# The first expert's rows are transposed ahead of the second search's counts, and that search's first levels move into the expert's phase

## The reference

```python
def _moe2_ref(x, w_gate, w1, w2) -> np.ndarray:
    N, D = x.shape                 # 3072, 384
    E = w_gate.shape[1]            # 8
    cap = N // E                   # 384
    logits = x @ w_gate
    flat = logits.flatten()
    order = np.argsort(-flat)
    ...
    for idx in order:
        tok, e = (int(idx) // E, int(idx) % E)
        if assigned[tok] >= 0 or counts[e] >= cap:
            continue
        assigned[tok] = e
        counts[e] += 1
    ...
    for e in range(E):
        mask = assigned == e
        h = np.maximum(x[mask] @ w1[e], 0.0)      # 384 x 1024
        out[mask] = h @ w2[e]
```

## Time and profile before

| | |
|---|---|
| runs before | 803.28, 801.63, 803.12 us; median 803.12 |
| profiled execution | 805.37 us, its span 803.3 us |
| PE busy | 785.6 us, 98% of the span |
| DVE busy | 537.0 us, 67% |
| search 0's `slots` on PE | begins at 539.49 us |
| phase 0 begins (n = 0) | 549.21 us |
| the chain that ended last | PE 90%, DMA 4%, DVE 2% |

### The profile page before, as it was taken

One profiled execution on the slowest core, in us unless ns is written; L12 is line 12 of the kernel. 1 busy time (PEld: TensorE's weight loads), 2 busy tenths in 40 slices (PEclk: granted clock), 3 DMA queues, 4 the chain that ended last, 5 costly groups with the idle time before them and its releaser, 6 DMA issues.

```text
span 803.3 us, 16845 instructions
## 1 busy us (share of the span) xinstructions
PE 785.6 (98%) x6663; PEld 654.2 (81%) x6663; DVE 537.0 (67%) x1280; ACT 273.4 (34%) x511; POOL 175.8 (22%) x169
## 2 busy tenths in 40 slices
PE   8799999999999999999999999989999999999996
PEld 5677777777777877777777888668999999999996
DVE  7887767776677776777776545665867757667321
ACT  3443324433433343334434444311222122122321
POOL 5523142212222222222120040001122221231211
PEclk9999999999999999999999999999999999999999
DMA  8734225666666666666675566327467466564950
GB/s 265 247 135 135 83 95 184 224 214 207 200 208 215 206 205 220 214 214 221 214 260 170 173 215 212 137 70 287 163 229 262 169 224 218 222 250 144 341 218 29
DMA packets 62910, 158.72 MB, mean 198 GB/s; under 512 B 8304, under 2 KB 11632, under 8 KB 62832
## 3 DMA queue, kind: packets, MB, share of 16 engines
q1 hardware_dynamic: 56880, 144.28, 53.2%
q0 software_dynamic: 3072, 9.44, 3.6%
q10 hardware_dynamic: 2880, 3.93, 1.3%
HBM read 106.24 MB, written 51.38 MB: 196 GB/s over the span
## 4 chain that ended last, share of the span: by engine, by line
PE 90%; DMA 4%; DVE 2%; issue 1%; SPq 1%; ACT 0%; POOL 0%; POOLq 0%; DVEq 0%
PE ACC L1534 25%; PE U L1508 24%; PE ACC L1727 13%; PE U L1714 13%; DMA stage<-in_dw 3%; PE P L1625 3%; PE P L1391 3%; PE P L1408 2%; PE P L1478 2%; PE P L1400 1%; PE ACC L1571 1%; PE P L1490 1%; DMA WL<-split_low 1%; PE P L1650 1%; PE P L1452 0%
## 5 line engine op out<-in xcount | busy, mean ns | idle before, releaser
L1010 DVE TENSOR_TENSOR hr<-hr 128x512 f32<-128x512 f32 x96 | 67.9, 707 | 80.9 <-ACT hr L774 80.7
L1508 PE MATMUL U<-XH,WH 128*128 128x512 f32 x285 | 113.4, 398 | 0.0
L1508 PE MATMUL U<-XH,WL 128*128 128x512 f32 x285 | 112.9, 396 | 0.0
L1508 PE MATMUL U<-XL,WH 128*128 128x512 f32 x285 | 112.9, 396 | 0.0
L774 ACT ACTIVATE hr<-U 128x512 f32<-128x512 f32 x96 | 57.3, 596 | 162.0 <-PE U L1508 160.0
L1534 PE MATMUL ACC<-HH,WH 128*128 128x512 f32 x252 | 105.6, 419 | 2.7 <-DVE HL L1024 2.7
L1534 PE MATMUL ACC<-HL,WH 128*128 128x512 f32 x252 | 99.9, 397 | 0.0
L1534 PE MATMUL ACC<-HH,WL 128*128 128x512 f32 x252 | 99.8, 396 | 0.0
L1040 DVE TENSOR_TENSOR stage<-stage 128x512 fp32r<-128x512 f32 x80 | 68.8, 861 | 26.2 <-ACT stage L754 23.9
L886 ACT ACTIVATE HH<-U 128x384 fp32r<-128x384 f32 x64 | 31.5, 492 | 145.3 <-PE U L1714 142.3
L754 ACT ACTIVATE HH<-hr 128x512 fp32r<-128x512 f32 x84 | 53.1, 632 | 77.2 <-DVE hr L1010 77.2
(11 more groups left out here) (252 smaller groups left out, 1472.2 us busy)
## 6 DMA issues: line engine op xcount, KB each, us to landing
stage<-in_ew SPq DMA_DIRECT2D x80, 256.0 KB, 3.6
split_high<-stage SPq DMA_DIRECT2D x80, 256.0 KB, 2.1
split_low<-stage SPq DMA_DIRECT2D x80, 256.0 KB, 2.5
WH<-split_high SPq DMA_DIRECT2D x40, 512.0 KB, 5.9
WL<-split_low SPq DMA_DIRECT2D x40, 512.0 KB, 6.6
tok<-in_tok SPq DMA_DIRECT2D x24, 640.0 KB, 7.0
rk<-in_rk SPq DMA_DIRECT2D x22, 448.0 KB, 5.8
stage<-in_dw SPq DMA_DIRECT2D x8, 768.0 KB, 7.8
```

The costliest lines, as they stand in the source:

```text
L1010: tt(hr[:, s % 2, :], hr[:, s % 2, :], hr[:, s % 2, :], ALU.mult).then_inc(sq_done, 1)
L1508: ins = mm(U[s % 2][:, :], w_up((WH, WL)[a], k, s), (XH, XL)[b][:, q, k, :], start=(n == 0), stop=(n == 3 * KT - 1))
```

## The change

It does three things. PE's program between search 0 and phase 0: 80 matmuls of 128 columns go, ten of 512 columns and later two more stand in their place; the transposes of block 0 stand ahead of the count of level 0; the digit of level 0 and the count of level 1 leave this stretch. The tables of phases 0 and 1: search 1's levels 0 and 1 become visits of phase 0, with all that follows up to `slots` 13 places later; search 2's level 1 moves from the end of phase 0 to the start of phase 1, with what follows 10 places later. DVE's order: blocks 0 and 1 are split ahead of `filled(1, 0)`, and block 2 ahead of `descend(1, 0)`; in phase 0 the next rows are split ahead of `filled(2, 0)`.

```diff
+        TURN_0 = [(134, "row", 1, 0), (134, "row", 1, 1), (137, "row", 1, 2), (140, "count", 2, 0), (143, "digit", 2, 0)]
+
+        def later(by, plan):
+            return [(at + by, *what) for at, *what in plan]
+
         def visits(k):
...
             if k == 0:
-                return [(2, "digit", 1, 1)] + LEVELS + CHOICE + TURN
+                return ([(2, "digit", 1, 0), (12, "count", 1, 1), (17, "digit", 1, 1)] + later(13, LEVELS)
+                        + later(13, CHOICE) + TURN_0)
+            if k == 1:
+                return [(5, "count", 1, 1), (11, "digit", 1, 1)] + later(10, LEVELS) + later(10, CHOICE) + TURN
             return LEVELS + CHOICE + (TURN if k < NE - 3 else TURN_5)
...
             compare(0)
+            split_rows(0, 0)
+            split_rows(0, 1)
             filled(1, 0)
+            split_rows(0, 2)
             descend(1, 0)
-            for j in range(CB):
-                split_rows(0, j)
             filled(1, 1)
...
                     low_part(k, 7)
+                    if k == 0:
+                        for j in range(CB):
+                            split_rows(r, j)
                     filled(r + 1, 0)
                     descend(r + 1, 0)
-                    for j in range(CB):
-                        split_rows(r, j)
+                    if k > 0:
+                        for j in range(CB):
+                            split_rows(r, j)
                     filled(r + 1, 1)
...
             slots(0)
-            warm_up(6 * STIR, P[0])
-            count(1, 0)
-            digit_of(1, 0)
-            warm_up(STIR, P[0])
+            keep_warm(10, P[0])
             pe.wait_ge(row_done, NT)
             transpose_rows(0, 0)
-            warm_up(STIR, ACC[2])
+            count(1, 0)
             transpose_rows(0, 1)
-            count(1, 1)
+            keep_warm(2, ACC[2])
             transpose_rows(0, 2)
-            warm_up(STIR, ACC[2])
```

## The result

The changed kernel is slower: 812.0 us (811.44 to 812.29, four runs) against 802.38 us (800.85 to 803.28, four runs) of the kernel before, a ratio of 1.0121 with an interval of 1.0102 to 1.0140. That is 9.6 us, where 6.3 were forecast. The median lies at the very end of the range, 812, and the change is larger than the forecast by half.

A forecast was written before the change was run, and what follows sets the result against it. PE, busy 98% of the span, bounds the kernel with a full queue through the eight phases. 0 up to n = 27, 2.0 in phase 0, 3.6 in phase 1 and 0.7 for the clock give +6.3 us: 809.4 us, range 806.7 to 812.

The forecast's parts named there:

- The start: Seam before phase 0: tile 0's second part starts at 550.0 instead of 551.15, so n = 9 gains 1.14 us.
- Where it goes: Phase 0 up to n = 27: a count (0.81 us), a 1.5 us wait at n = 18 and piece 3's landing take the gain.
- `slots` too late in phase 0: Phase 0: `slots(1)` moves from n = 94 to 107, so n = 126 waits 2.0 us for `low_part(0, 6)`.
- Phase 1: Phase 1: a count and digit (0.9 us) plus waits of 0.55, 0.45 and 1.7 us cost 3.6 us.
- the clock's 0.7 us: Seam: idle PE lets the clock fall to half once; the part behind 548.3 costs 0.7 us, bounds 0 and 2.5.
- the landings don't change: Seam: the gathers' issue does not change, so they land when they did; piece 3 of the weights likewise.
- n = 27 stands where it stood: Phase 0: PE reaches n = 27 at 557.3, as piece 3 lands; up to there the change gains and costs nothing.
- The sum: Whole kernel: 0 up to n = 27, 2.0 in phase 0, 3.6 in phase 1, 0.7 clock: +6.3 us, median 809.4.
- The clock stays up: Rival at the seam: no fall of the clock, so +5.6 us, 808.7 us; chance 0.23.
- The low parts are in time: Rival in phases 0 and 1: DVE's waits vanish, only phase 1's 0.9 us is paid, 804.0 us; chance 0.05.
- That a gain needs weights to land earlier: Rival at n = 27: a real gain, 1.1 us or more, needs piece 3 to land earlier too; chance 0.02.

## Why the prediction was wrong in size, point by point

- **The start** was right: the second part of tile 0 follows the split, and n = 9 gains 1.0 us (1.14 forecast).
- **Where it goes** was right in kind: one count, and the wait at n = 18 (1.33 us measured, 1.5 forecast).
- **`slots` too late in phase 0** was right: 1.85 us measured, 2.0 forecast; and moving the low part takes it away, the closed-up table takes it down to 0.8.
- **Phase 1** was right: 0.39, 0.29 and 1.55 us, where 0.55, 0.45 and 1.7 were forecast. Counted from start to start, as the forecast does, all five waits come within 0.02 us of it: 1.5, 2.0, 0.54, 0.45 and 1.7. All visits and waits behind n = 27 come to 5.84 us, 5.6 forecast.
- **The step that failed is the seam's: the clock's 0.7 us, and with it the sentences that the landings don't change and that n = 27 stands where it stood.** What the runs showed: the seam takes 18.3 to 20.6 us in six traces of the ten-filler order, 19.2 in the mean, against 17.9 and 18.2 before: 1.1 us in place of 0.7. The third transposes begin 9.0 to 9.9 us behind `slots`, 9.4 in the mean, against 8.8 and 9.3: some 0.3 us later, in numbers that overlap. From there to n = 27 PE took 9.3 to 9.5 us in the four traces with neither a wait for weights nor a long fall, where 9.0 was forecast. In one trace the weights came 1.1 us later than PE. And in one of the six the clock stayed down for 10.2 us, which cost 1.8; in four it fell for 3.4 us, which cost little, and in one it did not fall. A second fall, in phase 1, which the prediction did not have, stands in two of the five traces that have the wait of 1.55 us unfilled, and costs 1.6.
- **The sum.** 5.84 for n = 27 to own(3), 1.1 for the seam: 6.9 us; the two pairs of traces of these kernels show 7.0 and 7.9 up to own(3). The remaining 2.7 of the 9.6 are in timed executions of which there is no trace. The changed kernel's second trace, with one fall at the seam and none before it, is of an execution of 809.0 us with a mean clock of 0.996; the median of its ten runs is 812.0, at 0.991: 0.005 x 810 / 0.5 = 8 us more at half clock, or two to three falls of 3.4 us (an estimate; the clocks are rounded). Over the ten, the time follows the clock: 809.0 us at 0.996, 809.8 and 812.3 at 0.993, 811.4 to 812.0 at 0.991, 812.8 and 816.1 at 0.990, 815.1 at 0.988. With all new waits filled the clock was 0.997 to 0.999 and the median 3.3 to 3.6 us lower. So the missing time goes with the clock; in which stretch of which execution it falls, and how much of what the fillers gave back is the earlier gather instead, stays open.
- **The rivals.** "The clock stays up" is near what the run with all waits filled shows (808.7 was forecast for it, and 808.75 measured; that they agree so well is luck, since the fillers made the gather land sooner as well, and 808.7 was counted from a median 0.7 us higher). "The low parts are in time" needs other tables; with them the kernel was some 4 us slower (1.0046), not 0.9 as that rival had it, since the moved count is still paid and the seam is no shorter. That a gain needs weights to land earlier was right, and in the one way tried they delay the gathers by more. One thing in it was off: the early start meets piece 1 at n = 18 before it meets piece 3.

## What to carry to other kernels

A step that is moved out of a wait into a full stretch is paid twice: its own time, and the time by which everything chained to it comes late against the deadlines that didn't move (here 0.9 and 4.7 us behind n = 27). Ask of each moved step which wait of the other engine is queued behind it. And a wait of TensorE should be priced with its clock: with matmuls on constants in all the new waits the median was 3.3 to 3.6 us lower, of which the traces put 1.3 to 1.6 down to an earlier landing.

## What was not expected of the hardware

With 24 fillers ahead of the first transposes, the third gather's transposes began 8.2 us behind `slots` in each of three traces; with ten, 9.0 to 9.9 in six, and 8.8 to 9.3 with the old order in four. POOL issued the three gathers at the same distances in all (2.0, 3.5 to 3.7 and 4.9 to 5.1 us). So the last rows were there about a microsecond sooner with 24 fillers. That PE is busy is not enough to explain it: with the old order PE waits only 0.3 and 0.4 us ahead of the first transposes, and the third still begin at 8.8 to 9.3. No run was made to find out why.
